# The high parts of the output weights ahead of the gated value's; two pooled pairs scaled on ScalarE in the head; block 0's weights split as they come

## What is computed

```python
# attention, B=4, H=8, S=576, D=64, factor 4
q_d, k_d, v_d = means over 4 neighbouring rows          # pooled: 144 rows
out_d   = softmax(q_d @ k_d.T / 8) @ v_d ; out_up = repeat(out_d, 4)
scores  = where(|i - j| < 4, q @ k.T / 8, -1e9)         # a band of 7
out     = out_up + softmax(scores) @ v                  # -> x, 2304 x 512
# gated projection, d_ff = 1536
y = ((x @ w_a) * (x @ w_b)) @ w_out                     # 512 -> 1536 -> 512
# SoLU and LayerNorm, d_ff = 1024
h = y @ w_in ; t = h * softmax(h) ; ln = (t - mean) / sqrt(var + 1e-6) * g_ln
result = ln @ w_out2
```

## Time and profile before

| what | value |
| --- | --- |
| time, median of 3 runs | 782.8 us (780.17 to 783.48) |
| the profiled execution's own time | 782.83 us |
| its span | 781.0 us |
| TensorE busy | 760.9 us, 97% of the span |
| VectorE busy | 553.3 us (71%) |
| ScalarE busy | 300.2 us (38%) |
| POOL busy | 195.2 us (25%) |
| granted TensorE clock, mean | 0.998 of full |

### The profile page before, as it was taken

One profiled execution on the slowest core, in us unless ns is written; L12 is line 12 of the kernel. 1 busy time (PEld: TensorE's weight loads), 2 busy tenths in 40 slices (PEclk: granted clock), 3 DMA queues, 4 the chain that ended last, 5 costly groups with the idle time before them and its releaser, 6 DMA issues.

```text
span 781.0 us, 12653 instructions
## 1 busy us (share of the span) xinstructions
PE 760.9 (97%) x4626; PEld 703.5 (90%) x4626; DVE 553.3 (71%) x982; ACT 300.2 (38%) x819; POOL 195.2 (25%) x236
## 2 busy tenths in 40 slices
PE   8998899997999999999999999999999999999998
PEld 7888898997999999989999999999988888888886
DVE  5899978987868797877777876022367766666663
ACT  4646446462443525353424434234422222222222
POOL 3339776166434030060001212111100000000000
PEclk9999999999999999999999999999999999999999
DMA  9999936686888575482746523636121011011011
GB/s 183 217 208 231 212 107 195 193 232 185 253 199 238 150 197 167 146 234 67 210 142 186 134 89 112 216 98 225 43 68 55 28 54 55 28 55 54 28 41 40
DMA packets 94650, 108.84 MB, mean 139 GB/s; under 512 B 29309, under 2 KB 62589, under 8 KB 94589
## 3 DMA queue, kind: packets, MB, share of 16 engines
q1 hardware_dynamic: 83293, 99.38, 48.1%
q10 hardware_dynamic: 11296, 8.65, 3.7%
HBM read 87.46 MB, written 20.55 MB: 138 GB/s over the span
## 4 chain that ended last, share of the span: by engine, by line
PE 81%; POOL 6%; DVE 5%; DMA 2%; issue 2%; SPq 2%; ACT 2%; ACTq 0%; DVEq 0%
PE psum L940 25%; PE psum L942 24%; PE psum L941 24%; POOL raw L1830 2%; PE psum L1067 2%; POOL raw L1837 2%; PE psum L849 1%; POOL wo_lo L1857 1%; PE psum L897 1%; POOL w_lo L1849 1%; PE psum L873 1%; PE psum L908 1%; DVE tmp L1539 1%; DMA raw<-in_q 1%; DMA v_h<-in_v 1%
## 5 line engine op out<-in xcount | busy, mean ns | idle before, releaser
L940 PE MATMUL psum<-x_hi,w_hi 128*128 128x384 f32 x576 | 198.1, 344 | 3.1 <-POOL w_lo L1849 2.8
L942 PE MATMUL psum<-x_hi,w_lo 128*128 128x384 f32 x576 | 193.0, 335 | 0.0
L941 PE MATMUL psum<-x_lo,w_hi 128*128 128x384 f32 x576 | 192.8, 335 | 0.0
L940 PEld LDWEIGHTS psum<-x_hi,w_hi 128*128 128x128 f32 x576 | 108.2, 188 | 6.6 <-POOL w_lo L1849 3.5
L941 PEld LDWEIGHTS psum<-x_lo,w_hi 128*128 128x128 f32 x576 | 108.3, 188 | 0.0
L942 PEld LDWEIGHTS psum<-x_hi,w_lo 128*128 128x128 f32 x576 | 108.1, 188 | 0.0
L940 PE MATMUL psum<-ab_hi,wo_hi 128*128 128x384 f32 x288 | 100.4, 349 | 4.5 <-POOL wo_lo L1857 4.3
L942 PE MATMUL psum<-ab_hi,wo_lo 128*128 128x384 f32 x288 | 97.0, 337 | 0.0
L941 PE MATMUL psum<-ab_lo,wo_hi 128*128 128x384 f32 x288 | 96.9, 337 | 0.0
L1505 DVE TENSOR_TENSOR ab_f<-psum,a_sb 128x384 f32<-128x384 f32 x72 | 39.9, 554 | 78.1 <-PE psum L942 52.6
L1233 ACT ACTIVATE a_sb<-psum 128x384 f32<-128x384 f32 x72 | 35.3, 490 | 107.7 <-PE psum L942 107.7
(11 more groups left out here) (159 smaller groups left out, 1431.5 us busy)
## 6 DMA issues: line engine op xcount, KB each, us to landing
wo_hi<-wo_hi_scratch SPq DMA_DIRECT2D x53, 256.0 KB, 2.7
wo_lo<-wo_lo_scratch SPq DMA_DIRECT2D x53, 256.0 KB, 3.1
wo_raw<-in_moe_w_out SPq DMA_DIRECT2D x19, 256.0 KB, 5.2
yT_scratch<-y_sb ACTq DMA_DIRECT2D x6, 768.0 KB, 4.2
y_raw<-yT_scratch SPq DMA_DIRECT2D x18, 256.0 KB, 2.9
out<-out_sb SPq DMA_DIRECT2D x18, 256.0 KB, 2.1
k_u<-in_k SPq DMA_DIRECT2D x11, 384.0 KB
v_u<-in_v SPq DMA_DIRECT2D x11, 384.0 KB
```

What stands on the lines that cost most here:

```text
L940: mm(dst, wh, xh, start=first, stop=False, skip_group_check=not check)
L941: mm(dst, wh, xl, start=False, stop=False, skip_group_check=not check)
L942: last = mm(dst, wl, xh, start=False, stop=end, skip_group_check=not check)
```

## The change

It has seven parts.

1. On ScalarE, in every step, `wo_high(g+1)` stands directly ahead of `ab_high(g+1)`; before, it stood behind it and behind the unit work of the step's last third.
2. On POOL, in step 3 of tile 0, `wo_low(4)` stands ahead of `pool_sums(1, 2, 1)`; before, behind it.
3. Block 11 of `w_a` and `w_b` is split in step 7 of tile 0 in place of step 8, on ScalarE and on POOL.
4. In the head ScalarE scales the pooled pairs 2 and 3 (`head_pooled_scale`: a copy with a factor for each row, two per pair); VectorE only makes the reciprocal for them.
5. The first block's `w_a` has a semaphore of its own (`wa_loaded`). ScalarE makes its high part as soon as it is there (`first_high`), and that of `w_b` after two of the four `x_high` (`second_high`); before, one instruction waited for both.
6. VectorE does `head_x(2)` ahead of `x_low(0, 0)` and `head_x(3)` ahead of `x_low(0, 1)`.
7. TensorE and `weight_low(0, WA)` wait for the new semaphores.

The diff, without the list of semaphore names:

```diff
-SPLIT_AT = {0: (2,), 2: (4,), 3: (5,), 4: (6,), 5: (7, 8), 6: (9, 10), 8: (11,)}
+SPLIT_AT = {0: (2,), 2: (4,), 3: (5,), 4: (6,), 5: (7, 8), 6: (9, 10), 7: (11,)}
...
-                                     src[hh][:, :, 2 * i * 128:(2 * i + 2) * 128]).then_inc(w_loaded[i], 16)
+                                     src[hh][:, :, 2 * i * 128:(2 * i + 2) * 128]
+                                     ).then_inc(s.wa_loaded if i == 0 and kind == WA else w_loaded[i], 16)
...
             def head_turn_pooled(c):
-                pe.wait_ge(s.hp_normed, c + 1)
+                if c < 2:
+                    pe.wait_ge(s.hp_normed, c + 1)
+                else:
+                    pe.wait_ge(s.hp_normed_by_scalar, c - 1)
...
+            def head_pooled_scale(c):
+                act.wait_ge(s.hp_inv_ready, c - 1)
+                for h in range(2):
+                    last = A(p_head[:, c, h, :], p_head[:, c, h, :], ACT.Copy, scale=hp_inv[:, c, h:h + 1])
+                last.then_inc(s.hp_normed_by_scalar, 1)
...
             def weight_high(j):
-                act.wait_ge(w_loaded[j // 2], 64)
+                if j < 2:
+                    act.wait_ge(s.wa_loaded, 32)
+                act.wait_ge(w_loaded[j // 2], 32 if j < 2 else 64)
                 A(w_both(w_hi, j), w_both(w_raw, j), ACT.Copy).then_inc(s.w_hi_ready, 1)
+            def first_high():
+                act.wait_ge(s.wa_loaded, 32)
+                A(w_part(w_hi, WA, 0), w_part(w_raw, WA, 0), ACT.Copy).then_inc(s.wa_hi_ready, 1)
+            def second_high():
+                act.wait_ge(w_loaded[0], 32)
+                A(w_part(w_hi, WB, 0), w_part(w_raw, WB, 0), ACT.Copy).then_inc(s.w_hi_ready, 1)
...
             head_pooled_exp(3)
-            weight_high(0)
+            head_pooled_scale(2)
+            head_pooled_scale(3)
+            first_high()
             head_pooled_pT(2)
             head_pooled_pT(3)
             x_high(0, 0)
             x_high(0, 1)
+            second_high()
...
                     from_tensor(m, 3 * j + 2)
+                    if g > 0 and g + 1 < FC * TILES and wo_fresh(g + 1):
+                        wo_high(g + 1)
                     if g + 1 < FC * TILES:
                         ab_high(g + 1)
                     of_units(m, 3 * j + 2)
-                    if g > 0 and g + 1 < FC * TILES and wo_fresh(g + 1):
-                        wo_high(g + 1)
...
+                if c >= 2:
+                    V.reciprocal(hp_inv[:, c, :], hp_den[:, c, :]).then_inc(s.hp_inv_ready, 1)
+                    return
...
             head_x(1)
+            head_x(2)
             x_low(0, 0)
-            head_x(2)
+            head_x(3)
             x_low(0, 1)
-            head_x(3)
...
+                    if g > 0 and g + 1 < FC * TILES and wo_fresh(g + 1):
+                        wo_low(g + 1)
                     if m == 0 and j == 3:
                         pool_sums(1, 2, 1)
-                    if g > 0 and g + 1 < FC * TILES and wo_fresh(g + 1):
-                        wo_low(g + 1)
```

More of the change, by code:

```diff
@@ L392, in build_program @@
         h_turned qT_by_vector qT_by_scalar kT_ready kd_ready qd_summed qd_ready h_scored h_masked h_exped h_inv_ready h_normed h_p_turned h_pT_ready h_x_mm
-        hp_scored hp_bias_ready hp_exped hp_normed hp_turned hp_pT_ready
+        hp_scored hp_bias_ready hp_exped hp_inv_ready hp_normed hp_normed_by_scalar hp_turned hp_pT_ready
         h_up_mm x_local x_summed
@@ L397, in build_program @@
         loc_chain k_used v_used q_used u_sub_ready u_exped u_normed u_act_values acc_ready x_turned x_hi_ready x_lo_ready
-        w_hi_ready w_lo_by_vector w_lo_by_pool wo_hi_ready wo_lo_by_vector wo_lo_by_pool
+        wa_loaded wa_hi_ready w_hi_ready w_lo_by_vector w_lo_by_pool wo_hi_ready wo_lo_by_vector wo_lo_by_pool
         a_mm a_copied b_mm ab_ready ab_hi_ready ab_lo_by_vector ab_lo_by_pool y_mm y_copied
@@ L1481, in weight_low @@
             def weight_low(j, kind):
-                dve.wait_ge(s.w_hi_ready, j + 1)
+                if j == 0 and kind == WA:
+                    dve.wait_ge(s.wa_hi_ready, 1)
+                else:
+                    dve.wait_ge(s.w_hi_ready, j + 1)
                 V.tensor_tensor(w_part(w_lo, kind, j), w_part(w_raw, kind, j), w_part(w_hi, kind, j), ALU.subtract
```

## The result

The changed kernel takes 777.0 us, the median of seven runs (774.79 to 780.48), against 782.5 us for the kernel before beside it (seven runs, 780.17 to 784.54). The profile shown is of an execution of 780.48 us, the slowest of the seven, with a span of 778.7 us; it must be read with its clock in view.

The account below looks back on a forecast made before the run. TensorE, busy 97% of the span, was taken as the bound, gaining only where it stands still, chiefly for POOL. Terms 2.1 - 0.5 + 0.5 + 0 = 2.1 us took 782.8 to 780.7 us, range 778.0 to 783.0.

Parts of the forecast that it names:

- POOL in tile 0: Tile 0, 76 to 84 us: `wo_low(4)` ends at 81.25, down(4) starts at 81.4 and not 83.48; 2.1 us gained.
- as long as VectorE is in such work: POOL in tile 0: its work costs the same wherever moved beside VectorE; `wo_low(4)` stays 2.83 us, gain 2.1, otherwise 2.6.
- I take the landing as fixed: Tile 0: `wo_raw(3)` still lands at 66.9 us, DMA being full, so 0.5 of POOL's 2.8 us is left.
- `ab_high` behind `wo_high`: ACT at 101.21 us: `ab_hi` comes 0.5 us later, so `accT` at 132.44 does too; 0.5 us lost.
- Block 11 a step earlier: Tile 0, steps 7 and 8: most of the 1.27 us wait at 124.09 goes, PE waits elsewhere; gain nothing, cost nothing.
- the next thing PE needs is `accT` at 132.44, which VectorE sets: End of tile 0: VectorE sets PE's next need, so splitting block 11 earlier gains nothing and costs nothing.
- The head: PE reaches up(0) at 36.6, some 0.4 us earlier, but POOL sets the time at 76 us; 0 kept.
- Tile 1: Waits of 0.52 and 1.67 us at 176.64 and 185.83 go; only the first is kept, 0.5 us gained.
- The second is not: Tile 1: the 1.67 us is lost at `accT` (194.34), held by `xup` loads after a store; wait grows 2.01 to 3.7.
- a sign of being wrong: Tile 1: if the wait before `accT` stays at 2 us, the forecast is wrong and 1.7 us more is gained.
- Rival (a): More is kept: earlier `wo_raw(3)` (1.3 us) and tile 1's `xup` loads (1.2 us), 4.6 us in all, 778.2; chance 0.20.
- The sum: Whole kernel: 2.1 - 0.5 + 0.5 + 0 = 2.1 us gained, 780.7 us.

Follow-up runs that it names:

- the new table: Kernel before with `wo_high` ahead of `ab_high` in both tiles and block 11 split in step 7 (SPLIT_AT 7 for 8): 776.72 us, 0.9932.
- Tile 0 alone: Kernel before with `wo_high(g+1)` ahead of `ab_high(g+1)` in tile 0 only, tile 1 as before: 783.28 us, 1.0004.
- tile 1 alone: Kernel before with `wo_high(g+1)` ahead of `ab_high(g+1)` in tile 1 only, tile 0 as before: 778.65 us, 0.9956.
- filling the stop of the tile-0 kernel: Kernel before with `wo_high` ahead in tile 0 only, plus ten unused identity products in PE's stop ahead of up(5): 781.40 us, 0.9987.
- The changed kernel with the loads of `xup` first: Changed kernel with the two loads of `xup` ahead of `store_wo(16)` on SP: 776.56 us, 0.9901.
- all three edits: Changed kernel with `xup` loads ahead of block 16's store, `load_wo(3)` ahead of `load_weights(3)`, and ten identity products ahead of up(5): 775.82 us, 0.9924.

## Why the prediction was wrong

**"POOL in tile 0", 2.1 us gained.** Right in POOL's times to 0.1 us, in an execution where the transfer landed as assumed. Wrong in how they come about. The prediction has 0.5 us from the earlier start and 1.6 from putting `wo_low(4)` ahead of `pool_sums`, and held that POOL's work costs the same wherever it is moved "as long as VectorE is in such work". But with `wo_high` ahead alone, `pool_sums` still first, PE takes 76.29 us from up(0) to the first pooled scores against 78.45 before, at full clock: 2.2 us, where the terms give 0.5 (75.87 with the new table too). Part 2 in its turn gave POOL 0.1 to 0.9 us and not 1.6. There `wo_low(4)` took 1.41 us, and a VectorE instruction stood for 6.88 us beside it. So which of the two engines pays is not fixed by both being at work; it changed from one profile to another. Nor is the gain there in every execution. PE takes 78.84 us in the changed kernel's own profile, where the clock fell, and 78.35 where `wo_raw(3)` came late. "I take the landing as fixed" was a second weak step: counted from up(0), ACT took `wo_raw(3)` off its transfer 29.9 us later in the profile of before, and 28.6 to 31.4 us later in the others in which it waited for it; that spread is larger than the gain. Tile 0 alone, without part 2, measured no gain (1.0004).

**"`ab_high` behind `wo_high`", 0.5 lost.** Right: 16.97 us before, 17.41 with that part alone, 0.44 lost in the stretch it was put in.

**"Block 11 a step earlier", nothing.** Wrong as to the stretch, by 0.7 us (49.40 to 48.74 from down(4) to `accT`). The step "the next thing PE needs is `accT` at 132.44, which VectorE sets" was true, but VectorE's time for it was taken as given. POOL's work was moved from beside VectorE's last adds to a place ahead of them, and they ran at 0.95 us and not at 1.49. In whole time the part is not shown: 0.9932 with it and 0.9933 without.

**"The head", 0 kept.** Nothing speaks against it: 0.9993 alone. PE reached up(0) at 36.73 in the profile after, as forecast (36.6), but at 37.08 with the head alone (37.02 before).

**"Tile 1", 0.5 gained.** This is the step that failed. "The second is not [kept]", since VectorE stood "for the loads of `xup` ... which follow the store issued at 184.74". The store's end at 187.22 and the loads' issue at 187.16 in the profile of before only fell together; these loads do not wait for that store, and in fact they came out of SP's queue behind a store that waited for POOL. POOL came 3.96 us earlier (0.73 of it brought along from tile 0, 2.0 by its own shorter instructions), and the stretch between the two `accT` shrank by 2.88 us in the profile after (61.90 to 59.02), 3.54 with tile 1 alone, 2.47 with `wo_high` alone; in time tile 1 alone gave 0.9956, 3.4 us. So 3 us or so stood in place of 0.5, and the wait did not grow to 3.7 but is 1.76, which the prediction itself had named as a sign of being wrong, at 1.7 us more. Rival (a) had the right sign and named SP's queue, with 1.2 us for it, and 0.20 of the chance.

**The sum again**, by stretches at full clock with what was measured: 2.2 - 0.4 + 0.7 + 0 + 2.9 = 5.4 us, against 5.1 measured (2.9 to 7.4). The first term comes from single profiles at full clock (78.45 to 76.29, and 76.20 for the change without the head) and is the least sure, since the clock and the landing of `wo_raw(3)` can take it; that the sum comes so near is in part luck.

**Open.** That long stops bring the clock down near 75 us is what the profiles go together with, and filling the stop of the tile-0 kernel kept it up; what it is worth in time is below what these runs resolve (about 2 us). What makes VectorE and not POOL stand in some profiles near 80 us was not tested. Why part 1 alone gives the ratio of the whole change, although the stretches say that part 3 adds 0.7 us, is not settled: the interval on each ratio is about 2 us to either side. The changed kernel with the loads of `xup` first has the lowest ratio, 0.9901, but its interval (0.9862 to 0.9939) takes in the changed kernel's 0.9935; the version with all three edits, 0.9924, is no better.

## What to carry to other kernels

A time that falls together with another in a profile is not what released it: ask which instructions stand ahead in the same queue, what each of these waits for, and follow that chain, in the program's text too; here a load of one tensor hung on the low part of another, two instructions ahead on SP. When work is moved from beside an engine that sets the end, cost the neighbour's faster or slower instructions too, not only the slots. And a gain at a stop that ends on a transfer beside full DMA engines is worth a range from nothing to its size, since the landing moves by more than the gain.

## What was not expected of the hardware

A stop of PE seems to cost more than its length. Executions of one program differ by up to 10 us (before: 778.6 to 788.9 in the 108 executions of the four sets of comparisons), and the granted clock goes with it: over 275 executions of these kernels, each compared with those of its own kernel, 0.001 more of mean granted clock goes with 0.6 us less. The Trainium skill (TensorE: Matmul & The Clock Gate, What's actually happening) says that the clock is gated to half after idleness and released by activity; the windows at 74 to 82 us agree. The falls are not tied to one place: with all three edits the clock is full there, but it falls to half from 97 to 103 us, after PE had waited 0.74 and 1.20 us for raw k rows at 91.6 and 95.7.

A VectorE instruction can stand for several times its length beside a busy POOL. A multiplication of 128x768 that takes 0.94 us alone stood for 6.88 us with `wo_high` alone, while POOL's instructions kept their short times:

```profile
78.45 6.88 DVE L1579 TENSOR_TENSOR part<-v_u,p_u 128x768 f32<-128x768 f32 x1
```

```profile
79.65 1.41 POOL L1857 TENSOR_TENSOR wo_lo<-wo_raw,wo_hi 128x256 fp32r<-128x256 f32 x2
```

Before, the same POOL instructions took 2.83 us, and the same VectorE instruction 1.63.
